# Keeping g, the masked scores and the attention output in PSUM, with 48-query windows and a written-out block 0

## What is computed

```
q_d, k_d, v_d = means over 4 neighbouring tokens        # 144 pooled tokens
out_d     = softmax(q_d k_d^T / 8) v_d, repeated 4 times
mask      = |i - j| < 4                                 # a band, 7 keys wide
out_local = softmax(where(mask, q k^T / 8, -1e9)) v
x = (out_d repeated + out_local) as [2304 tokens, 512]
h = x @ w_in            # w_in  512 x 2048
g = h * tanh(softplus(h))      # "Mish"
out = g @ w_out         # w_out 2048 x 512
```

## Time and profile before

| | |
|---|---|
| median of 3 runs | 509.79 us (509.51 to 510.77) |
| profiled execution, its own time | 509.98 us |
| its span, first to last instruction | 508.2 us |
| mean granted TensorE clock | 0.993 |
| PE busy | 487.1 us (96%) |
| DVE busy | 238.5 us (47%) |
| ACT busy | 180.8 us (36%) |
| POOL busy | 127.2 us (25%) |
| the chain that ended last | PE 78%, DVE 11%, issue 4%, POOL 3%, DMA 2%, ACT 2% |

### The profile page before, as it was taken

How to read it: one execution, slowest core, us unless ns; L and a number is a source line. 1 busy time by engine, 2 the same in 40 slices (tenths; PEclk the granted TensorE clock), 3 DMA queues, 4 the chain that set the end, 5 groups by cost and what they waited for, 6 DMA issues and landing times.

```text
span 508.2 us, 9125 instructions
## 1 busy us (share of the span) xinstructions
PE 487.1 (96%) x3748; PEld 431.9 (85%) x3748; DVE 238.5 (47%) x464; ACT 180.8 (36%) x384; POOL 127.2 (25%) x164
## 2 busy tenths in 40 slices
PE   7778898999999999999999999999999999999997
PEld 6667776887899998898898888989899999999996
DVE  4879995986422224476363555635322222222220
ACT  4685745636221114454343354434121111211111
POOL 4997644543100002051341313412000000000000
PEclk9899998999999999999999999999999999999999
DMA  8998130220200001323021150210010000100001
GB/s 285 297 308 283 54 90 21 77 74 27 78 35 0 1 0 49 96 66 98 4 94 50 50 154 12 94 50 1 1 63 0 1 0 2 41 22 0 1 0 62
DMA packets 15641, 33.58 MB, mean 66 GB/s; under 512 B 1776, under 2 KB 1904, under 8 KB 15600
## 3 DMA queue, kind: packets, MB, share of 16 engines
q1 hardware_dynamic: 15600, 33.00, 20.7%
HBM read 28.28 MB, written 4.72 MB: 65 GB/s over the span
## 4 chain that ended last, share of the span: by engine, by line
PE 78%; DVE 11%; issue 4%; POOL 3%; DMA 2%; ACT 2%; SPq 0%; POOLq 0%; ACTq 0%; DVEq 0%
PE acc L570 36%; PE hidden L553 33%; DVE w_out_low L747 2%; PE att L454 2%; PE att L441 1%; DMA k_t<-in_k 1%; DVE x_low L729 1%; PE att L516 1%; DVE g_high L740 1%; PE att L501 1%; POOL prob L369 1%; PE att L483 1%; PE att L472 1%; DMA out<-stage 1%; POOL prob_pool L377 1%
## 5 line engine op out<-in xcount | busy, mean ns | idle before, releaser
L740 DVE CAST g_high<-g_full 128x384 fp32r<-128x384 f32 x96 | 40.9, 426 | 197.3 <-PE acc L570 157.6
L553 PE MATMUL hidden<-x_high,w_in_high 128*128 128x384 f32 x384 | 131.1, 341 | 1.1 <-DVE x_low L729 1.1
L878 ACT ACTIVATE g_full<-hidden 128x384 f32<-128x384 f32 x96 | 47.2, 492 | 236.9 <-PE hidden L553 236.4
L553 PE MATMUL hidden<-x_high,w_in_low 128*128 128x384 f32 x384 | 130.1, 339 | 0.0
L553 PE MATMUL hidden<-x_low,w_in_high 128*128 128x384 f32 x384 | 129.4, 337 | 0.0
L570 PE MATMUL acc<-w_out_high,g_high 128*128 128x512 f32 x288 | 114.8, 399 | 2.4 <-DVE w_out_low L747 2.4
L570 PE MATMUL acc<-w_out_high,g_low 128*128 128x512 f32 x288 | 113.4, 394 | 0.0
L570 PE MATMUL acc<-w_out_low,g_high 128*128 128x512 f32 x288 | 113.3, 394 | 0.0
L553 PEld LDWEIGHTS hidden<-x_high,w_in_high 128*128 128x128 f32 x384 | 72.5, 189 | 6.1 <-DVE x_low L729 1.4
L553 PEld LDWEIGHTS hidden<-x_low,w_in_high 128*128 128x128 f32 x384 | 72.5, 189 | 3.1
L553 PEld LDWEIGHTS hidden<-x_high,w_in_low 128*128 128x128 f32 x384 | 72.5, 189 | 0.0
(11 more groups left out here) (100 smaller groups left out, 484.4 us busy)
## 6 DMA issues: line engine op xcount, KB each, us to landing
v_win<-in_v_win SPq DMA_DIRECT2D x16, 320.0 KB
q_t<-in_q SPq DMA_DIRECT2D x16, 296.0 KB, 3.1
k_t<-in_k SPq DMA_DIRECT2D x16, 296.0 KB, 4.2
v_in<-in_v SPq DMA_DIRECT2D x16, 288.0 KB
out<-stage SPq DMA_DIRECT2D x17, 256.0 KB, 2.1
w_in_raw<-in_w_in SPq DMA_DIRECT2D x16, 256.0 KB, 12.2
w_out_raw<-in_w_out SPq DMA_DIRECT2D x16, 256.0 KB, 6.2
out<-last_stage SPq DMA_DIRECT2D x1, 256.0 KB, 2.1
```

The source lines that it names most:

```text
L553: last = nc.tensor.matmul(hidden[:, g % HB, 0:TB], w, x[:, k, cols], start=(k == 0 and i == 0), stop=(k == KT - 1 and i == 2))
L740: nc.vector.tensor_copy(g_high[:, g % GB], g_full[:, g % 2]).then_inc(g_rounded, 1)
L878: nc.scalar.activation(g_full[:, g % 2], hidden[:, g % HB, 0:TB], ACT.Mish).then_inc(mish_ready, 1)
```

## The change

- **g in place.** `mish` writes g over h in the `hidden` bank, and `split_g` reads it there with both of its instructions. `first_product` of slice g now waits for `g_split` of slice g - 2, where it waited for `mish_ready`. `mish` no longer waits for a free buffer.
- **Attention in place.** For pairs 4 to 15 the mask is added in `att` itself, the maxima are taken there, and one subtraction writes the shifted scores to SBUF (before: mask addition to SBUF in two instructions, then maxima and subtraction in SBUF). `upsample` copies 144 numbers a row, not 576; `combine` is one instruction in place in PSUM, which reads each of them four times; `round_x` and `split_x` read PSUM. The bank is then in use until `split_x`, so the next pair's `band_scores` and `outputs` wait for `x_split`, where they waited for `combined`.
- **Windows.** 48 queries by 54 keys, exactly twelve windows: 24 small score matmuls a pair for 20, 6 transposes for 5, 24 output matmuls for 20. The v windows are 768 numbers a partition for 640, and the pooled v input has 80 rows for 72 (8 of them unused).
- **Block 0 and the start.** Every engine's order there is written out call by call; the loop begins at block 1.

```diff
-WQ = WK - 2 * REACH
-W = -(-S // WQ)
+WQ = 48
+KW = WQ + 2 * REACH
+W = S // WQ
 T = W // 2
+TP = T // 2
+WT = 2 * WQ
...
-        Q_IN, K_IN, V_IN, V_WIN = [P, COLS], [P, COLS], [GH, 2, POOL, 2 * D], [P, 2 * T * D]
+        mask = const[:, P:P + T * KW]
+
+        Q_IN, K_IN, V_IN, V_WIN = [P, S], [P, COLS], [VR, 2, POOL, 2 * D], [P, 2 * T * D]
...
-        def x_of(n):
-            return x_home if n >= AHEAD else (x_even, x_odd[:])[n % 2]
+        def pooled_out(n):
+            return sets[0]["prob"][:].rearrange("p w k -> p (w k)")[:, 0:G] if n >= AHEAD else stage[:, n % 2, 0:G]
...
+        def x_out(n):
+            return out_bank(n)[:, 0:2, 0:S // 2]
...
+                sp.dma_start(const[:], const_l).then_inc(const_loaded, 16)
                 load_qk(0)
-                sp.dma_start(const[:], const_l).then_inc(const_loaded, 16)
                 load_qk(1)
+                load_w_out(0)
+                load_w_in(0)
...
                 pool_q(0)
                 pool_q(1)
-                pool_v(0)
+                low_in(0)
                 pool_q(2)
                 normalize_band(0)
                 normalize_pooled(0)
-                pool_v(1)
+                pool_v(0)
...
-                        pe.wait_ge(combined, n)
+                        pe.wait_ge(x_split, split(n - 1))
...
-                                    att[WK * c:WK * (c + 1), h, WK * t:WK * (t + 1)],
-                                    q_t[rows, at:at + WK], k_t[rows, PAD - REACH + at:PAD - REACH + at + WK],
+                                    att[WK * c:WK * c + WQ, h, KW * t:KW * (t + 1)],
+                                    q_t[rows, at:at + WQ], k_t[rows, PAD - REACH + at:PAD - REACH + at + KW],
...
-                    for tp in range(2):
+                        pe.wait_ge(x_split, split(n - 1))
+                    for tp in range(TP):
                         for c in range(2):
                             for r in range(2):
-                                keys = slice(WK * r, WK * (r + 1))
+                                keys = slice(WK * r, WK * r + KW)
...
                 def first_product(j, f, tiles=range(KT)):
                     g = FT * j + f
                     if g == 0 and tiles[0] == 0:
-                        pe.wait_ge(combined, AHEAD - 1)
+                        pe.wait_ge(x_split, split(AHEAD - 2))
                     if g >= HB:
-                        pe.wait_ge(mish_ready, g - HB + 1)
+                        pe.wait_ge(g_split, g - HB + 1)
...
+                first_product(0, 0, range(KT - 1, KT))
+                first_product(0, 1, range(KT - 1, KT))
+                first_product(0, 2)
+                second_product(0, 0)
...
+                    s, scores = work(n), band_scores_of(att)
                     dve.wait_ge(band_scored, n + 1)
+                    if n >= AHEAD:
+                        dve.wait_ge(const_loaded, 16)
+                        masked_scores = att[:, 0:2, 0:T * KW]
+                        nc.vector.tensor_tensor(
+                            masked_scores, masked_scores,
+                            mask.rearrange("p (o k) -> p o k", o=1).broadcast_to([P, 2, T * KW]),
+                            ALU.add).then_inc(masked, 1)
+                        dve.wait_ge(masked, n - AHEAD + 1)
+                    top = s["top"][:, 0:W].rearrange("p (h t) -> p h t", h=2)
+                    nc.vector.tensor_reduce(top, scores, AX_X, ALU.max).then_inc(band_top, 1)
+                    dve.wait_ge(band_top, n + 1)
...
+                        windows(s).rearrange("p (h t) k -> p h t k", h=2), scores,
+                        top.rearrange("p h (t o) -> p h t o", o=1).broadcast_to([P, 2, T, KW]),
                         ALU.subtract).then_inc(shifted, 1)
...
                 def combine(n):
-                    b, x = out_bank(n), x_of(n)
                     dve.wait_ge(up_ready, n + 1)
-                    main = x[:, 0:8 * WQ].rearrange("p (t r i) -> p r t i", r=2, i=2 * WQ)
-                    nc.vector.tensor_tensor(main, b[:, 0:2, 0:4 * WQ].rearrange("p r (t i) -> p r t i", i=2 * WQ),
-                                            main, ALU.add).then_inc(main_combined, 1)
-                    for h in range(2):
-                        rows = slice(D * h, D * (h + 1))
-                        last = nc.vector.tensor_tensor(
-                            x[rows, 8 * WQ:S], b[rows, h, 4 * WQ:4 * WQ + S - 8 * WQ], x[rows, 8 * WQ:S], ALU.add)
-                    last.then_inc(combined, 1)
+                    x = x_out(n).rearrange("p r (g o) -> p r g o", o=POOL)
+                    up = pooled_out(n).rearrange("p (r g o) -> p r g o", r=2, o=1).broadcast_to([P, 2, G // 2, POOL])
+                    nc.vector.tensor_tensor(x, x, up, ALU.add).then_inc(combined, 1)
...
+                    x = x_out(n).rearrange("p r (t i) -> p r t i", i=WT)
+                    high, low = tokens(x_high[:, k, cols].bitcast(F32)), tokens(x_low[:, k, cols])
+                    for part in (slice(0, 2), slice(2, TP)) if n == AHEAD - 1 else (slice(0, TP),):
+                        nc.vector.tensor_tensor(low[:, :, part], x[:, :, part], high[:, :, part],
                                                 ALU.subtract).then_inc(x_split, 1)
...
-                    nc.vector.tensor_copy(g_high[:, g % GB], g_full[:, g % 2]).then_inc(g_rounded, 1)
+                    x = hidden[:, g % HB, 0:TB]
+                    nc.vector.tensor_copy(g_high[:, g % GB], x).then_inc(g_rounded, 1)
                     dve.wait_ge(g_rounded, g + 1)
-                    nc.vector.tensor_tensor(g_low[:, g % GB], g_full[:, g % 2], g_high[:, g % GB].bitcast(F32),
+                    nc.vector.tensor_tensor(g_low[:, g % GB], x, g_high[:, g % GB].bitcast(F32),
                                             ALU.subtract).then_inc(g_split, 1)
...
-                        act.wait_ge(x_split, split(n - 2))
-                    nc.scalar.activation(
-                        x_of(n).rearrange("p (g r) -> p g r", r=POOL),
-                        out_bank(n)[:, 1, OUT_POOL].rearrange("p (g o) -> p g o", o=1).broadcast_to([P, G, POOL]),
-                        ACT.Copy, scale=1.0 / POOL).then_inc(up_ready, 1)
+                        act.wait_ge(combined, n - 1)
+                    nc.scalar.activation(pooled_out(n), out_bank(n)[:, 1, OUT_POOL], ACT.Copy,
+                                         scale=1.0 / POOL).then_inc(up_ready, 1)
...
-                    nc.scalar.copy(x_high[:, k, cols], x_of(n)).then_inc(x_rounded, 1)
+                    nc.scalar.copy(tokens(x_high[:, k, cols]), x_out(n).rearrange("p r (t i) -> p r t i", i=WT)
+                                   ).then_inc(x_rounded, 1)
...
                 def mish(g):
                     act.wait_ge(hidden_ready, g + 1)
-                    if g >= 2:
-                        act.wait_ge(g_split, g - 1)
-                    nc.scalar.activation(g_full[:, g % 2], hidden[:, g % HB, 0:TB], ACT.Mish).then_inc(mish_ready, 1)
+                    x = hidden[:, g % HB, 0:TB]
+                    nc.scalar.activation(x, x, ACT.Mish).then_inc(mish_ready, 1)
...
+    v_in_l = _np.zeros((PAIRS, VR, 2 * POOL * 2 * D), _np.float32)
+    v_in_l[:, 0:GH] = v.reshape(PAIRS, 2, 2, GH, POOL, D).transpose(0, 3, 2, 4, 1, 5).reshape(
+        PAIRS, GH, 2 * POOL * 2 * D)
```

467 lines of the change are left out of this document (307 added, 160 removed).

## The result

The changed kernel is slower: 514.21 us median of 12 runs (510.02 to 518.85) against 509.95 of 12 of the kernel before, run beside it; ratio 1.0077, 95% interval 1.0055 to 1.0100. I had forecast 502.0 and a range that ends at 508.5. The highest of the twelve was an execution in the chip's slower state; without it the highest is 516.91 and the median 514.19, and the ratio is of those eleven. The profiled execution took 511.93 us, at the low end of its runs: 2.3 us under the median, so its stages add up to less than what a usual execution loses.

What follows compares the result with a forecast made beforehand. TensorE was taken to set the time behind 132.24 us, all engines' chain before it. Start -2.2, block 0 -8.4, x_split +2.4 and windows +0.4 sum to -7.8: 502.0 us against 509.79, range 498.0 to 508.5.

Steps and rivals of the forecast that it cites:

- Part 5: Start: the first product comes at 37.3 us, after pair 3's pool_v on GpSimd: -2.2 us (bounds -3.0 and +1.5).
- Part 6: Block 0: 5.0 us of waits for 13.4, of which 2.8 from stretched low_out: -8.4 us (bounds -11.2 and +8.6).
- the walk: Block 0's written order: TensorE waits 1.2 us at slice 2, 0.4 at slice 7, 0.6 at pair 7's scores.
- B: Rival: half of block 0's waits stay (6.7 us) and the start gains only 0.7: 505.2 us; chance 0.14.
- D: Rival: slower; each of block 0's 14 first products waits for split_g, at 1.3 us each 517 us; chance 0.09.
- Part 3: Behind block 0, band_scores waits for x_split: 1.05 us at each of two pairs, 0.3 at six others; +2.4 us.
- Part 4: Windows, behind block 0: more but smaller matmuls cost 0.05 us a pair, +0.4 us over eight pairs.
- parts 1 and 2: Subtractions from PSUM take 554 ns and no longer stretch beside GpSimd; the wait for g_split costs 0 in blocks 1 to 5.
- The named signs: Among them: g_low near 555 ns, g_high near 550, low_out still stretched, block 1's first product 10 to 11 us earlier.
- the sign by which I said that I would be wrong: Wrong if block 0's TensorE waits for g_low sum over 5 us, or the start ends no earlier than 39.

Runs made afterwards that it cites:

- e4: The kernel before with the changed kernel's written-out call lists on every engine and none of its new parts; 511.84 us, ratio 1.0050.
- e6: The changed kernel with eleven more idle matmuls on TensorE ahead of pair 1's pooled scores; 514.72 us, ratio 1.0103.
- e7: The changed kernel with pooled_maxima(0) moved right behind band_maxima(0) on VectorE; 515.05 us, ratio 1.0097.
- e1: The changed kernel with the old call lists in the start and block 0, split_x of pairs 0 and 1 ahead of the next combine; 522.88 us, ratio 1.0233.
- e11: The changed kernel with x back in SBUF and the old call lists in the start and block 0; 507.57 us, ratio 0.9962.
- e10: The changed kernel with x back in SBUF, so that the output bank's next users wait for combined, not x_split; 513.17 us, ratio 1.0076.
- e9: The changed kernel with low_out(1) moved on VectorE from ahead of split_g(0) to behind split_g(2); 508.88 us, ratio 0.9985.
- e15: The kernel before with the changed kernel's call lists, and low_out(1) behind split_g(2); 510.49 us, ratio 1.0016.
- e3: The changed kernel with the old call lists in block 0 and the new ones in the start; 511.34 us, ratio 1.0035.
- e5: The changed kernel with g written to SBUF again, first_product waiting for mish_ready alone; 512.61 us, ratio 1.0060.
- e8: The changed kernel with the loads of w_in from slice 4 on held until three pairs' outputs are done; 514.90 us, ratio 1.0106.
- e14: The changed kernel with x in SBUF, old start lists, low_out(0) behind split_g(0) and low_out(1) behind split_g(2); 507.11 us, ratio 0.9946.
- e17: e13 with waits on GpSimd: low_in(4) for split_x(3), low_in(5) to (7) for the splits of g of slices 0 to 2; 508.09 us, ratio 0.9973.
- e18: e16 with GpSimd's low_in(2) and (3) waiting for split_x(2) and (3), low_in(4) to (6) for splits of g; 509.95 us, ratio 1.0016.
- e13: The changed kernel with x in SBUF and low_out(1) behind split_g(2); 512.02 us, ratio 1.0041.
- e16: e13 with low_out(0) moved behind split_g(0) and pooled_maxima(0) right behind band_maxima(0) on VectorE; 507.44 us, ratio 0.9973.

## Why the prediction was wrong

**Part 5 (the start) failed, in sign.** The step that failed is its first: that pair 3's `pool_v` on GpSimd is the last thing that the outputs of pair 3 need, so that GpSimd's work prices the start. `pool_v`(3) ended at 39.13 us, 2.9 later than I had it, and still well before TensorE began the outputs of pair 3, at 41.92: it was not what the start waited for. It was not so in the kernel before either. There `pool_v`(3) ended at 36.33, and TensorE began these outputs at 38.04 and their pooled part at 38.89:

```profile
38.04 0.69 PE L501 MATMUL acc<-prob_t,v_win 64*64 64x58 f32 x32
...
38.89 0.72 PE L516 MATMUL acc<-prob_pool_t,v_pool 72*64 72x144 f32 x8
```

What ends the changed kernel's start is TensorE's own list and what holds it up. The chain that ended last (start us, us, what) runs over VectorE and ScalarE to the wait of 3.60 us; from 14.56 to 43.51 it is TensorE's list, but for 1.1 us in ScalarE's copies and the issue gaps:

```profile
13.23 1.20 ACT prob_pool L944 x6
14.43 0.14 issue
14.56 1.73 PE att L489 x6
...
34.07 1.90 issue
35.98 0.78 PE hidden L535 x35
```

I walked neither. The new lists alone lengthen the start by 2.0 us (e4). The forecast's own upper bound, +1.5, is below even this. e4 has the same wait (3.58 us), which stands in VectorE's list for anyone to read. But the wait alone is not the loss: up to pair 0's transposes TensorE waited 4.4 us in the kernel before as well, in four pieces, and 4.5 in the changed one. What differs is the work done by then: pair 1's pooled scores and pair 2's band scores ended at 12.7 and 15.7 us in the kernel before, and now begin at 14.56 and 18.04, behind the wait and at a granted clock of 0.50 (12.8 to 19.6 us). Whether the clock costs the start anything isn't shown, since e6 kept it up there and e7 took the wait apart, and neither start got shorter by more than the scatter. The hold of the bank I had at nothing in the start; e1 and e11 show that it is 12.6 us with the old lists, and e10 that the new ones hide it. Of the +3.87, then, some 2 are the order, and about 1 to 2 the other parts together with the scatter of a start; which of them, stays open. Two smaller ones: 36.8 with 1.45 us of slow issue is 38.3 and not 38.7, and the changed start has not 1.45 us of such gaps but 3.38.

**Part 6 (block 0): the sum of the waits came out in the profile, the base under them and the place of the stretch did not.** The 84.3 was 79.3 of undisturbed work and 5.0 of waits. The profiled execution has 4.5 us of TensorE idle and 83.5 of work. e9, whose granted clock is 1.00 throughout block 0, shows the work more cleanly (columns as in the earlier trace rows):

```profile
42.96:128.22 85.26, 81.93 (x763) 71.93 (x762) 58.69 (x99) 48.00 (x103) 38.16 (x44) 1.00 0.33 103
```

That is 3.3 us idle and 81.9 of work, 2.6 more than the pace of block 1 gave. So e9's 85.26 beside the 84.3 is partly luck: the 2.8 us of stretching that the sum let through are not in e9, and the base was short by about as much. For the same reason not all of the 13.4 us could be won from waits: TensorE was idle for 8.3 us in the kernel before (92.70 less 84.41). Of the walk's places, slice 2 and pair 7's scores wait as walked (1.2 and 0.5 us); slice 7 waits 1.44 for 0.4:

```profile
48.65 0.45 PE L580 MATMUL hidden<-x_high,w_in_high 128*128 128x384 f32 x1 [1.23 <-DVE g_low L809]
...
73.67 0.45 PE L580 MATMUL hidden<-x_high,w_in_high 128*128 128x384 f32 x1 [1.44 <-DVE g_low L809]
```

The larger loss is the stretch. I added 2.8 us of stretched `low_out` as a mean over block 0, and did not ask which `low_out` stands ahead of a split that TensorE waits for. It was `low_out`(1), beside three or four `low_in` in a row: 3.2 to 6.0 us, and about 5 us of the kernel's time (e9). I also had the reason of the gain half wrong: the order alone gives nothing (e4, e15), the parts give 5.7 (e3). In the upper bound, the 9.1 us of stretching on L742 are of the whole run; 6.4 of them lie in block 0.

**The rivals.** B had the mechanism and its size (3 to 4 us on the first products), on pair 4's bias instruction ahead of `combine`(3). That very instruction took 3.2 us in e5, e6 and e8, and 5.35 in e14, where it stands ahead of `split_g`(0); in the changed kernel's profile it took 0.63, and `low_out`(1) did the harm. B had the start gain 0.7 all the same. D forecast a slower kernel, but by a wait at each of 14 first products: two waited for `g_low`, 4.0 us in sum. Its 517 also leaves out the 2.8 us of the rest; 502.0 and 18.2 are 520.

**Part 3 (x_split): right in mechanism and place, short in size.** TensorE waited ahead of pair 9's scores by 1.53 us where it had 0.42, and at pair 13's by 1.50 where it had 0.43: 1.1 each for the 1.05 worked out. In sum the hold costs 3.3 us (e10) for the 2.4 forecast, so the six other pairs pay about 0.2 each and not 0.05.

```profile
214.85 0.79 PE L476 MATMUL att<-k_t,q_t 64*48 64x54 f32 x48 [1.53 <-DVE x_low L795]
```

**Part 4 and the reads of PSUM (parts 1 and 2): right, slightly better.** Without the hold the rest takes 375.30 for 375.96: -0.7, where +0.4 was forecast for the windows and 0 for the wait for `g_split`. The two errors of the rest, +0.9 and -1.1, cancel in its sum: that it came out as forecast is luck.

**The named signs.** `g_low` 558 ns and `g_high` 556 held; so did `low_out` and pairs 9 and 13, and blocks 1, 4 and 5 changed by less than 0.1 us each. Block 1's first product came 0.9 us earlier, not 10 to 11. TensorE's waits for `g_low` were 4.0 us in the profiled execution, under the 5 that I had named, and 7.5 in e7. The start ended later than 39: the sign by which I said that I would be wrong.

## What to carry to other kernels

A subtraction of VectorE with all its data in SBUF, a copy there, or a `tensor_scalar` on a few columns lasted in these kernels until a row of GpSimd operations was over; so look, ahead of every instruction that TensorE waits for, at what stands before it on VectorE, and move that behind, or break GpSimd's row with a wait, if what it delays is not waited for in turn (e17 gained, e18 did not). A bank that is read in place is held longer: count who else uses the bank before counting the SBUF traffic saved. And a startup is a chain over several engines, so a new list for it has to be walked on all of them, as block 0 was here; no version tried beat the kernel before by more than 0.54% (e14, 0.31 to 0.77%), and that one keeps the old start.

## What the runs showed of the hardware

- The victim need not be large or have two inputs: in e14 a `tensor_scalar` of 3 columns took 5.35 us beside GpSimd's `low_in`, ahead of the first split of g. The splits of g, which read PSUM, kept to 0.54 to 0.56 us right behind it.

```profile
45.87 5.35 DVE L769 TENSOR_SCALAR small<-small 96x3 f32<-96x3 f32 x1
```

- Not every operation stretches. In all twenty traces no VectorE instruction that reads PSUM took over 0.84 us, no `tensor_reduce` out of SBUF over 0.83 and no `reciprocal` over 0.23; those that stretched are `tensor_tensor` with two inputs in SBUF, `tensor_scalar`, and the copy of g from SBUF (2.10 us in e15).
- The stretch ended with the row of `low_in`, not with GpSimd's work: in e13 that row ends at 50.70 us and `split_x`(3) at 51.32, while GpSimd had gone on with `pool_q` at 50.67.
- The stretch depends on where in GpSimd's row the operation begins: `low_out`(1) took 3.23, 5.51, 5.91, 5.92 and 5.96 us in five near copies. This is a likely reason for two clusters of times in e16; no single run shows it.
- TensorE's granted clock fell to its lower level, 1.2 GHz, in or behind stretches with little work for it (granted clock 0.50 from 12.8 to 19.6 us in the changed kernel, where a wait of 3.60 us ends at 14.56), and small matmuls took up to 1.8 times as long there (1.49 us for 0.82).
